# Loading three tiles' keys and queries in 32x32 squares and turning them on VectorE instead of TensorE

## The chip, the cores and the metric

One NeuronCore of a Trainium2 chip runs the whole program in one launch. The metric is the device time of one execution in microseconds (us), and the median of three runs stands for a kernel. The engines are TensorE (PE in the profile, its weight loads PEld), VectorE (DVE), ScalarE (ACT), GpSimd (POOL) and SyncE (SP), which here only issues DMAs. Each engine runs its own instruction list in order, and semaphores order the engines among each other.

## The reference: windowed attention, then two feed-forward stages

```python
# q, k, v: [2, 8, 768, 64] float32; sinks 4, window 128
scores = scale * q @ k.T; keep = (pos_k < 4) | (0 <= pos_q - pos_k < 128)
a = softmax(where(keep, scores, -1e9)); x = (a @ v) -> [1536, 512]
out = sum_e p[:, e] * (relu(x @ w1[e]) @ w2[e])   # 4 experts, F = 1024
h = out @ w_in; return (h * cos(h)) @ w_out       # d_ff = 2048
```

## The kernel before

The 1536 tokens are 12 tiles of 128 (`T` = 12, 6 for each batch), and the 8 heads make 4 pairs for each tile. The attention stage runs in rounds `i` = 0 to 26. Round `i` computes the scores of two head pairs, so tile `t` has its scores in rounds 2t and 2t+1. Each engine has its own loop over the rounds, written by hand, and that order is the order of its instructions. In round `i`:

- PE computes the scores of the round (`scores`, L1406), turns the weights of the round before (`turn_weights`, L1417), turns keys or queries of a tile that is needed later (`turn_keys` L1349 in odd rounds, `turn_queries` L1368 in even ones, four 128x128 transposes against the identity each), turns the sink weights with the sums (`turn_sinks` L1382, odd rounds) and multiplies weights with values three rounds late (`weigh_values` L1441, `weigh_sinks` L1455).
- DVE merges and masks the scores (`merge` L1042, `mask_head` L1058), copies turned keys out of PSUM (`copy_keys` L1069), for three tiles the queries too (`copy_queries` L1075, the tiles in `QUERIES_BY_DVE`), inverts the sums (L1087, L1091), and in rounds 18, 20, 21 and 23 makes one of four sums of the first batch's result for the feed-forward stage (`sum_tokens` L1129).
- ACT takes the exponentials (L779), copies turned weights (L787), the other tiles' queries (`copy_queries` L796) and the result (`copy_out` L768).
- POOL splits the sink weights (`gather_sinks`, L610 and L612, even rounds), parts the turned weights (`part_weights`, L595 and L598), copies sink keys (L630), makes low halves of expert weights (`first_lo` L665, in rounds 11, 13 and 15) and multiplies the result of tile `t` with its norms in round 2t+6 (`normalise` L651).
- SP has a loop over tiles, `t` = 1 to 12: two norm DMAs for tile t-3, keys of tile t+3, the store of tile t-2's inverse sums, queries of tile t+3, values of tile t. The norm DMAs read back, spread over 64 partitions each, what the store wrote (`load_norm` L436).

PE may be one pair ahead of the masks: `scores(j)` waits until the pair j-2 is masked. `turn_sinks(t)` waits for `gather_sinks(t)`, and `scores` of a tile waits for its keys and queries in `k_t` and `q_t`. From round 24 on the feed-forward products follow (three matmuls in fp32r for each fp32 product), some 750 us of them; they start when the masks are done and the first tokens are split. `turn_squares` (L1264) and `place_squares` (L472) of that stage already turn tiles with VectorE and small DMAs.

## Time and profile before

| | |
|---|---|
| median of 3 runs | 837.62 us (834.06 to 837.65) |
| profiled execution | 837.64 us, span 835.9 us |
| PE, DVE, ACT, POOL busy | 831.0, 455.7, 458.0, 551.7 us |
| granted TensorE clock | 1.00 in all 40 slices |
| DMA packets | 101045, 70.46 MB, 68368 of them under 512 B |

The profile is one execution. The span is what the engines' records cover, and the execution's own time is 1.7 us more. A busy PE is not a PE at its peak, since the ends of matmuls are modelled. In a timeline each row is a start, a length, and what ran; a bracket gives the idle time before it and who ended it.

### The profile page before, as it was taken

The numbers are of one execution on the slowest core, as the hardware profiler recorded it, in microseconds if no ns is written. First come the engines' busy times: TensorE is split into PE (matmuls) and PEld (weight loads), VectorE is DVE, ScalarE is ACT, GpSimd is POOL, SyncE is SP. The second block draws the span as 40 slices with busy tenths as digits, with TensorE's granted clock in tenths as the row PEclk, the third lists the DMA queues.
The fourth block names the chain that finished last, engine by engine and source line by source line (L and its number), as shares of the span: only waits on it lengthen the run. The fifth ranks groups of instructions, "written<-read, shape, count | busy, mean of one in ns | idle before, by whom it ended". The sixth has DMA issues, their size and how long they took to land.

```text
span 835.9 us, 13778 instructions
## 1 busy us (share of the span) xinstructions
PE 831.0 (99%) x4564; PEld 743.6 (89%) x4564; DVE 455.7 (55%) x947; ACT 458.0 (55%) x985; POOL 551.7 (66%) x417
## 2 busy tenths in 40 slices
PE   9999999999999999999999999999999999999998
PEld 7777989988988988988988998998998998998997
DVE  4988833523523427633433433338767749756756
ACT  5888734334334435433423523525867869867864
POOL 3777996476476778575475575878384399685450
PEclk9999999999999999999999999999999999999999
DMA  8785231211221220432331131130223430530202
GB/s 184 169 190 147 67 123 51 102 61 44 98 68 44 91 83 19 117 105 53 95 112 50 52 101 51 51 101 30 73 63 76 125 117 0 177 102 18 84 1 76
DMA packets 101045, 70.46 MB, mean 84 GB/s; under 512 B 68368, under 2 KB 74864, under 8 KB 100976
## 3 DMA queue, kind: packets, MB, share of 16 engines
q1 hardware_dynamic: 100976, 69.58, 28.5%
q8 instruction: 39, 0.64, 0.3%
q14 instruction: 30, 0.25, 0.1%
HBM read 62.96 MB, written 3.19 MB: 79 GB/s over the span
## 4 chain that ended last, share of the span: by engine, by line
PE 96%; DVE 1%; issue 1%; ACT 1%; DMA 0%; SPq 0%; ACTq 0%; DVEq 0%
PE scores L1499 11%; PE scores L1503 11%; PE scores L1501 11%; PE scores L1512 10%; PE scores L1514 10%; PE scores L1510 10%; PE bank L1512 5%; PE bank L1514 5%; PE bank L1510 5%; PE bank L1499 3%; PE bank L1501 3%; PE bank L1503 3%; PE scores L1406 2%; PE bank L1441 2%; PE bank L1417 1%
## 5 line engine op out<-in xcount | busy, mean ns | idle before, releaser
L665 POOL TENSOR_TENSOR w_lo<-w_raw,w_hi 128x512 fp32r<-128x512 f32 x96 | 129.8, 1362 | 139.0 <-ACT w_hi L814 139.0
L1499 PE MATMUL scores<-x_hi,w_hi 128*128 128x384 f32 x528 | 177.1, 335 | 0.4 <-DVE x_lo L1136 0.2
L1503 PE MATMUL scores<-x_hi,w_lo 128*128 128x384 f32 x528 | 176.8, 335 | 0.0
L1501 PE MATMUL scores<-x_lo,w_hi 128*128 128x384 f32 x528 | 176.5, 334 | 0.0
L672 POOL TENSOR_TENSOR w_lo<-w_raw,w_hi 128x1024 fp32r<-128x1024 f32 x48 | 116.2, 2431 | 65.4 <-ACT w_hi L824 65.4
L824 ACT ACTIVATE w_hi<-w_raw 128x1024 fp32r<-128x1024 f32 x48 | 50.9, 1060 | 190.2 <-PE scores L1514 188.8
L1514 PE MATMUL scores<-w_hi,h_lo 128*128 128x512 f32 x384 | 149.3, 389 | 0.0
L1512 PE MATMUL scores<-w_lo,h_hi 128*128 128x512 f32 x384 | 149.3, 389 | 0.0
L1510 PE MATMUL scores<-w_hi,h_hi 128*128 128x512 f32 x384 | 149.0, 388 | 0.0
L1240 DVE SCALAR_TENSOR_TENSOR acc<-scores,probs,acc 128x512 f32<-128x512 f32 x56 | 41.8, 749 | 116.5 <-PE scores L1514 116.5
L1499 PEld LDWEIGHTS scores<-x_hi,w_hi 128*128 128x128 f32 x528 | 99.1, 188 | 2.4 <-issue 0.7
L1501 PEld LDWEIGHTS scores<-x_lo,w_hi 128*128 128x128 f32 x528 | 99.1, 188 | 0.9
L1503 PEld LDWEIGHTS scores<-x_hi,w_lo 128*128 128x128 f32 x528 | 99.1, 188 | 0.0
L665 POOL TENSOR_TENSOR w_lo<-w_sum,w_hi 128x768 fp32r<-128x768 f32 x48 | 92.5, 1928 | 0.0
L1514 PEld LDWEIGHTS scores<-w_hi,h_lo 128*128 128x128 f32 x384 | 72.1, 188 | 14.9
L1510 PEld LDWEIGHTS scores<-w_hi,h_hi 128*128 128x128 f32 x384 | 72.1, 188 | 14.1
L1512 PEld LDWEIGHTS scores<-w_lo,h_hi 128*128 128x128 f32 x384 | 72.1, 188 | 14.0
L1512 PE MATMUL bank<-w_lo,h_hi 128*128 128x512 f32 (+1 forms) x196 | 76.0, 388 | 0.0
L1514 PE MATMUL bank<-w_hi,h_lo 128*128 128x512 f32 (+1 forms) x196 | 75.9, 387 | 0.0
L1510 PE MATMUL bank<-w_hi,h_hi 128*128 128x512 f32 (+1 forms) x196 | 75.8, 387 | 0.0
L660 POOL TENSOR_TENSOR w_sum<-w_raw 128x512 f32<-128x512 f32 x46 | 59.5, 1293 | 15.8 <-DMA w_raw<-in_moe_w_in_dram 13.6
L1204 DVE SCALAR_TENSOR_TENSOR h_lo<-scores,h_hi 128x384 fp32r<-128x384 f32 x64 | 35.5, 554 | 44.1 <-ACT h_hi L878 42.6
(140 smaller groups left out, 1548.0 us busy)
## 6 DMA issues: line engine op xcount, KB each, us to landing
w_raw<-in_moe_w_dram SPq DMA_DIRECT2D x30, 1024.0 KB, 5.1
w_raw<-in_moe_w_in_dram SPq DMA_DIRECT2D x8, 1024.0 KB, 5.0
w_raw<-in_moe_w_out_dram SPq DMA_DIRECT2D x8, 1024.0 KB, 5.4
v_nat<-in_v_dram SPq DMA_DIRECT2D x12, 256.0 KB, 4.0
norm<-routing_dram SPq DMA_DIRECT2D x24, 128.0 KB, 3.2
x_t<-t_sum SPq DMA_DIRECT2D x192, 16.0 KB, 1.9
k_nat<-in_k_dram SPq DMA_DIRECT2D x11, 256.0 KB, 3.8
q_nat<-in_q_dram SPq DMA_DIRECT2D x11, 256.0 KB, 3.6
```

The lines of the kernel that those rows point to most:

```text
L660: nc.gpsimd.tensor_tensor(*weight_sum(n)).then_inc(w1_summed, 1)
L665: nc.gpsimd.tensor_tensor(w1_slots(w1_lo, h % 2, part), w1_part(h % 2, part), w1_slots(w1_hi, h % 2, part).bitcast(F32), ALU.subtract)\
L672: nc.gpsimd.tensor_tensor(w2_lo[:, i::2], w2_raw[:, i::2], w2_hi[:, i::2].bitcast(F32), ALU.subtract)\
L824: nc.scalar.activation(w2_hi[:, i::2], w2_raw[:, i::2], ACT.Copy).then_inc(w2_hi_ready, 1)
L1204: nc.vector.scalar_tensor_tensor(h_part(h_lo, h % 2, c), c_source(h % 2, c), 0.0, h_part(h_hi, h % 2, c).bitcast(F32), ALU.max, ALU.subtract)\
L1240: kept_one = nc.vector.scalar_tensor_tensor(acc[:, n], down_bank[k][:], probs[:, n, e:e + 1], acc[:, n], ALU.mult, ALU.add)
L1499: nc.tensor.matmul(target[:, 0:HALF], w1_hi[:, i, slot, d], x_hi[:, n - 1, d], start=first and d == 0, stop=False, skip_group_check=True)
L1501: nc.tensor.matmul(target[:, 0:HALF], w1_hi[:, i, slot, d], x_lo[:, n - 1, d], start=False, stop=False, skip_group_check=True)
L1503: last = nc.tensor.matmul(target[:, 0:HALF], w1_lo[:, i, slot, d], x_hi[:, n - 1, d], start=False, stop=d == 1, skip_group_check=True)
L1510: nc.tensor.matmul(target[:, cols], h_hi[:, i, f, toks], w2_hi[:, c, cols], start=i == 0 and f == 0, stop=False, skip_group_check=True)
L1512: nc.tensor.matmul(target[:, cols], h_hi[:, i, f, toks], w2_lo[:, c, cols], start=False, stop=False, skip_group_check=True)
L1514: return nc.tensor.matmul(target[:, cols], h_lo[:, i, f, toks], w2_hi[:, c, cols], start=False, stop=i == 1 and f == 1, skip_group_check=True)
```

## The change

- The keys and queries of tiles 9, 10 and 11 (`SQUARED` = 9) are no longer loaded as rows and turned by PE. 16 DMAs for keys and 16 for queries (`load_squares`), each of 32 partitions with 12 runs of 32 floats (48 KB), put the 32x32 squares where a square-by-square turn on DVE leaves the wanted layout. Keys go to `k_squares`, a part of `x_t` that is not in use yet, queries to `q_squares`, which lies under `x_lo`. One semaphore counts all 16 DMAs of each, so the first turned tile waits for all of them.
- DVE turns them with one `transpose` for each tile and kind, at the places in its loop where it copied them, in rounds 15 to 20. PE loses `turn_keys` and `turn_queries` of these tiles.
- The queries of tile 1 are copied by DVE instead of ACT.
- The sums 0 and 1 of the first batch are made by POOL in rounds 17 and 19 instead of DVE in rounds 18 and 20.
- The inverse sums are kept in another order of heads (`sum_at`), so that each norm DMA reads 64 x 512 floats in one run for each partition instead of four runs.

```diff
-QUERIES_BY_DVE = (7, 8, 9)
+QUERIES_BY_DVE = (1, 7, 8)
...
+        def sum_at(h):
+            return h % 2 * PAIRS + h // 2
...
+            def load_squares(dst, src, first, last, signal):
+                for n in range(first, last):
+                    h, f = divmod(n, 2)
+                    p, r = divmod(h, 2)
+                    rows = slice((2 * r + f) * 32, (2 * r + f + 1) * 32)
+                    source = src[1, h, (SQUARED - TPB) * P:S, f * 32:(f + 1) * 32]
+                    sp.dma_start(dst[rows, p, :].rearrange("j (c i) -> j c i", i=32),
+                                 source.rearrange("(c j) i -> j c i", j=32)).then_inc(signal, 16)
...
-                if 5 <= t + 3 < T:
+                if 5 <= t + 3 < SQUARED:
                     load_keys(t + 3)
                 if t >= 2:
                     store_inverse(t - 2)
-                if 5 <= t + 3 < T:
+                if 5 <= t + 3 < SQUARED:
                     load_queries(t + 3)
                 if 3 <= t < T:
                     load_values(t)
+                if t == 2:
+                    load_squares(k_squares, k, 0, 4, k_squares_landed)
+                elif t == 3:
+                    load_squares(k_squares, k, 4, 10, k_squares_landed)
+                elif t == 4:
+                    load_squares(k_squares, k, 10, 16, k_squares_landed)
+                elif t == 5:
+                    load_squares(q_squares, q, 0, 6, q_squares_landed)
+                elif t == 6:
+                    load_squares(q_squares, q, 6, 12, q_squares_landed)
+                elif t == 7:
+                    load_squares(q_squares, q, 12, 16, q_squares_landed)
...
+                if i in (17, 19):
+                    sum_tokens(0, (17, 19).index(i))
...
+                    nc.vector.transpose(target, k_squares[:, :, n * P:(n + 1) * P]).then_inc(k_ready, 1)
...
+            def turn_queries(t):
+                dve.wait_ge(q_squares_landed, 16 * SQUARE_PARTS)
+                dve.wait_ge(scores_done, PAIRS * (t - 1))
+                n = t - SQUARED
+                nc.vector.transpose(q_t[:, t % 2], q_squares[:, :, n * P:(n + 1) * P]).then_inc(q_squares_ready, 1)
...
-                if i % 2 == 1 and (i + 3) // 2 < T:
+                if i % 2 == 1 and (i + 3) // 2 < SQUARED:
                     turn_keys((i + 3) // 2)
-                elif i >= 2 and i % 2 == 0 and i // 2 + 1 < T:
+                elif i >= 2 and i % 2 == 0 and i // 2 + 1 < SQUARED:
                     turn_queries(i // 2 + 1)
```

SP in its loop for tiles 5 and 6, before. L436 are the norm DMAs, L410, L428, L416 and L422 the keys, the inverse sums, the queries and the values:

```order
L436 DMA norm<-routing_dram 64x4x128 x2
L410 DMA k_nat<-in_k_dram 128x8x64
L428 DMA routing_dram<-inverse 8x128
L416 DMA q_nat<-in_q_dram 128x8x64
L422 DMA v_nat<-in_v_dram 128x8x64
```

The same five of the changed kernel (L466, L429, L457, L435, L451), with the squares behind them (L445):

```order
L466 DMA norm<-routing_dram 64x512 x2
L429 DMA k_nat<-in_k_dram 128x8x64
L457 DMA routing_dram<-inverse 8x128
L435 DMA q_nat<-in_q_dram 128x8x64
L451 DMA v_nat<-in_v_dram 128x8x64
L445 DMA x_t<-in_k_dram 32x12x32 x6
```

Each SP loop from tile 3 to tile 6 has six more DMAs between the values and the norms of the next one; tiles 2 and 7 have four more.

PE in rounds 15 and 16, before, from the turned weights of round 15 to the values of round 16 (L1349 turns the keys of tile 9, L1368 its queries):

```order
L1417 MATMUL bank<-ident,weights 128x128 x4
L1349 MATMUL bank<-ident,k_nat 128x128 x4
L1382 MATMUL bank<-ident,sink_w 8x128
L1441 MATMUL bank<-weights_t,v_nat 64x128 x4
L1406 MATMUL scores<-k_t,q_t 128x264 x4
L1417 MATMUL bank<-ident,weights 128x128 x4
L1368 MATMUL bank<-ident,q_nat 128x128 x4
L1441 MATMUL bank<-weights_t,v_nat 64x128 x4
```

The changed kernel there:

```order
L1479 MATMUL bank<-ident,weights 128x128 x4
L1441 MATMUL bank<-ident,sink_w 8x128
L1503 MATMUL bank<-weights_t,v_nat 64x128 x4
L1468 MATMUL scores<-k_t,q_t 128x264 x4
L1479 MATMUL bank<-ident,weights 128x128 x4
L1503 MATMUL bank<-weights_t,v_nat 64x128 x4
```

One group of four transposes is gone from each of the rounds 15 to 20.

DVE behind the masks of round 18, before: the sums' inversion and the first token sum (L1129):

```order
L1058 ISA neg_max 128x1
L1087 TENSOR_TENSOR row_sum<-row_sum,tiny 128x8
L1091 RECIPROCAL sink_w<-row_sum 128x8
L1129 TENSOR_TENSOR t_sum<-x_t 128x768
L1042 COPY_PREDICATED scores<-in_prev,scores 128x2x128
```

The changed kernel there, with the turn of tile 10's queries (L1132) ahead of the inversion:

```order
L1097 ISA neg_max 128x1
L1132 STREAM_TRANSPOSE q_t<-q_squares 128x512
L1143 TENSOR_TENSOR row_sum<-row_sum,tiny 128x8
L1147 RECIPROCAL sink_w<-row_sum 128x8
L1081 COPY_PREDICATED scores<-in_prev,scores 128x2x128
```

The token sum has left DVE's rounds 18 and 20, and a transpose has come in.

## Rows read from the trace of the kernel before

**Rows 1.** The page: the chain that ended last, by engine.

```profile
PE 96%; DVE 1%; issue 1%; ACT 1%; DMA 0%; SPq 0%; ACTq 0%; DVEq 0%
```

**Rows 2.** Stages: stretch, its length, busy PE, PEld, DVE, ACT, POOL; clock, DMA share, GB/s.

```profile
60.00:76.00 16.00, 16.00 (x162) 12.46 (x161) 13.96 (x64) 14.48 (x52) 12.58 (x22) 1.00 0.54 141
...
33.00:40.00 7.00, 7.00 (x75) 5.50 (x71) 6.49 (x28) 5.60 (x21) 6.91 (x10) 1.00 1.00 219
```

**Rows 3.** Timeline of PE: scores of rounds 17, 18, 21 (L1406), `turn_sinks(7)` (L1382).

```profile
61.03 1.16 PE L1406 MATMUL scores<-k_t,q_t 64*128 64x264 f32 x8
...
63.05 0.27 PE L1382 MATMUL bank<-ident,sink_w 128*104 128x128 f32 x1
...
64.28 1.16 PE L1406 MATMUL scores<-k_t,q_t 64*128 64x264 f32 x8
...
74.60 1.16 PE L1406 MATMUL scores<-k_t,q_t 64*128 64x264 f32 x8
```

**Rows 4.** The chain in order of time: start, us on the chain.

```profile
72.81 0.44 PE bank L1368 x4
```

**Rows 5.** Timeline of DVE, rounds 16 to 21.

```profile
59.09 0.43 DVE L1042 COPY_PREDICATED scores<-in_prev,scores 128x256 f32<-128x256 int32 x1
...
60.89 0.69 DVE L1075 COPY q_t<-bank 128x512 f32<-128x512 f32 x1
...
61.82 0.41 DVE L1042 COPY_PREDICATED scores<-in_prev,scores 128x256 f32<-128x256 int32 x1
...
65.04 0.43 DVE L1042 COPY_PREDICATED scores<-in_prev,scores 128x256 f32<-128x256 int32 x1 [0.24 <-PE scores L1406]
...
67.16 0.91 DVE L1129 TENSOR_TENSOR t_sum<-x_t 128x768 f32<-128x768 f32 x1
68.58 0.43 DVE L1042 COPY_PREDICATED scores<-in_prev,scores 128x256 f32<-128x256 int32 x1 [0.52 <-PE scores L1406]
...
75.37 0.43 DVE L1042 COPY_PREDICATED scores<-in_prev,scores 128x256 f32<-128x256 int32 x1 [0.52 <-PE scores L1406]
```

**Rows 6.** Groups of DVE after 130 us, shapes apart: the transposes.

```profile
L1264 DVE STREAM_TRANSPOSE t_sum<-acc 128x512 f32<-128x512 f32 x12 | 7.8, 686 | 0.0
```

**Rows 7.** Timeline of SP's queue: start, time that the issue took.

```profile
17.67 2.04 SPq L443 DMA_DIRECT2D w_raw<-in_moe_w_dram  x4
...
26.26 0.39 SPq L416 DMA_DIRECT2D q_nat<-in_q_dram  x1
...
29.78 1.62 SPq L410 DMA_DIRECT2D k_nat<-in_k_dram  x1
31.45 0.48 SPq L428 DMA_DIRECT2D routing_dram<-inverse  x1
...
35.46 0.60 SPq L410 DMA_DIRECT2D k_nat<-in_k_dram  x1
...
51.04 1.24 SPq L436 DMA_DIRECT2D norm<-routing_dram  x2
...
61.14 0.40 SPq L422 DMA_DIRECT2D v_nat<-in_v_dram  x1
...
341.36 20.66 SPq L472 DMA_DIRECT2D x_t<-t_sum  x32
```

**Rows 8.** DMA issues by tile: count, KB each, median us to landing.

```profile
norm<-routing_dram SPq DMA_DIRECT2D x24, 128.0 KB, 3.2
x_t<-t_sum SPq DMA_DIRECT2D x192, 16.0 KB, 1.9
```

**Rows 9.** Timeline of POOL, rounds 14 to 16: `normalise(4)`, `part_weights(14)`, `gather_sinks(7)`.

```profile
55.30 1.27 POOL L651 TENSOR_TENSOR x_t<-x_t,norm 128x512 f32<-128x512 f32 x1 [1.62 <-DMA norm<-routing_dram]
58.52 0.64 POOL L595 TENSOR_SCALAR_AFFINE_SELECT weights_t<-weights_t 128x512 f32<-128x512 f32 x1 [1.96 <-ACT weights_t L787]
...
61.06 0.24 POOL L610 CAST sink_w<-weights 128x64 fp32r<-128x64 f32 x1
61.39 0.25 POOL L612 TENSOR_TENSOR sink_w<-weights,sink_w 128x32 fp32r<-128x32 f32 x1
```

More of the change, by code:

```diff
@@ L51, in program @@
     ROUNDS = ND + VALUE_LAG
+    SQUARED = T - 3
+    SQUARE_PARTS = 2 * H
     KC = DM // P
@@ L110, in program @@
         x_hi = sb("x_hi", [P, 7, 2, HALF], F32R)
+        early = ExitStack()
+        sb("early_lo", [P, 2, 2, HALF], stack=early)
+        q_squares = sb("q_squares", [P, PAIRS, HALF], stack=early)
+        early.close()
         x_lo = sb("x_lo", [P, 7, 2, HALF], F32R)
@@ L300, in sums_in_memory @@
             at = t % TPB * rows
-            return routing[at:at + rows, :].rearrange("(p r s) e -> p r (s e)", p=PAIRS, r=2)
+            return routing[at:at + rows, :].rearrange("(h s) e -> h (s e)", h=H)
         def weights_of(s):
@@ L434, in load_norm @@
                     sp.wait_ge(x_ready, t - 1)
+                sums = sums_in_memory(t).rearrange("(r p) s -> r (p s)", r=2)
                 for r in range(2):
-                    sp.dma_start(norm[r * D:(r + 1) * D, t % 2],
-                                 sums_in_memory(t)[:, r].unsqueeze(0).broadcast_to([D, PAIRS, P]))\
-                        .then_inc(norm_landed[t % 2], 16)
+                    sp.dma_start(norm[r * D:(r + 1) * D, t % 2].rearrange("d p s -> d (p s)"),
+                                 sums[r].unsqueeze(0).broadcast_to([D, PAIRS * P])).then_inc(norm_landed[t % 2], 16)
             def load_parts(dst, n, first, signal):
@@ L792, in copy_queries @@
                 act.wait_ge(q_turned, t + 1)
-                if t >= 2:
-                    act.wait_ge(scores_done, PAIRS * (t - 1))
-                source = out_bank if t == 1 else turn_bank
-                nc.scalar.activation(q_t[:, t % 2], source[:].rearrange("p (k s) -> p k s", k=PAIRS), ACT.Copy)\
+                act.wait_ge(scores_done, PAIRS * (t - 1))
+                nc.scalar.activation(q_t[:, t % 2], turn_bank[:].rearrange("p (k s) -> p k s", k=PAIRS), ACT.Copy)\
                     .then_inc(q_ready, 1)
@@ L923, in _ @@
                     exp_head(i, 3)
-                if i >= 2 and i % 2 == 0 and i // 2 + 1 < T and i // 2 + 1 not in QUERIES_BY_DVE:
+                if i >= 2 and i % 2 == 0 and i // 2 + 1 < SQUARED and i // 2 + 1 not in QUERIES_BY_DVE:
                     copy_queries(i // 2 + 1)
@@ L1063, in copy_keys @@
             def copy_keys(t):
-                dve.wait_ge(k_turned, t + 1)
+                if t < SQUARED:
+                    dve.wait_ge(k_turned, t + 1)
+                else:
+                    dve.wait_ge(k_squares_landed, 16 * SQUARE_PARTS)
                 if t >= 3:
@@ L1068, in copy_keys @@
                     dve.wait_ge(k_sink_kept, (t - 3) // TPB + 1)
[L1069 to L1070 removed]
+                target = k_t[:, :, t % 3, 0:P]
+                if t < SQUARED:
+                    nc.vector.tensor_copy(target, turn_bank[:].rearrange("p (k s) -> p k s", k=PAIRS))\
+                        .then_inc(k_ready, 1)
+                else:
+                    n = t - SQUARED
+                    nc.vector.transpose(target, k_squares[:, :, n * P:(n + 1) * P]).then_inc(k_ready, 1)
             def copy_queries(t):
                 dve.wait_ge(q_turned, t + 1)
+                if t >= 2:
+                    dve.wait_ge(scores_done, PAIRS * (t - 1))
+                source = out_bank if t == 1 else turn_bank
+                nc.vector.tensor_copy(q_t[:, t % 2], source[:].rearrange("p (k s) -> p k s", k=PAIRS))\
+                    .then_inc(q_ready, 1)
+            def turn_queries(t):
+                dve.wait_ge(q_squares_landed, 16 * SQUARE_PARTS)
                 dve.wait_ge(scores_done, PAIRS * (t - 1))
[L1075 to L1076 removed]
+                n = t - SQUARED
+                nc.vector.transpose(q_t[:, t % 2], q_squares[:, :, n * P:(n + 1) * P]).then_inc(q_squares_ready, 1)
             def copy_sinks(t):
@@ L1123, in sum_tokens @@
             def sum_tokens(n):
-                if n == 0:
-                    dve.wait_ge(x_ready, TPB)
-                else:
-                    dve.wait_ge(x_summed, n)
+                dve.wait_ge(x_summed, n)
                 nc.vector.tensor_tensor(*token_sum(0, n)).then_inc(x_summed, 1)
@@ L1150, in _ @@
                     copy_keys(1)
+                if i == 1:
+                    copy_queries(1)
                 if i % 2 == 1 and (i + 3) // 2 < T:
                     copy_keys((i + 3) // 2)
-                elif i % 2 == 0 and i // 2 + 1 in QUERIES_BY_DVE:
+                elif i >= 2 and i % 2 == 0 and i // 2 + 1 in QUERIES_BY_DVE:
                     copy_queries(i // 2 + 1)
+                elif i % 2 == 0 and SQUARED <= i // 2 + 1 < T:
+                    turn_queries(i // 2 + 1)
                 if i % 2 == 0 and 0 <= (i - 2) // 2 < T:
@@ L1165, in _ @@
                     sum_weights(i - 7)
-                if i in (18, 20, 21, 23):
-                    sum_tokens((18, 20, 21, 23).index(i))
+                if i == 21:
+                    sum_tokens(2)
+                elif i == 23:
+                    sum_tokens(3)
                 if i == 22:
@@ L1390, in scores @@
                 else:
-                    pe.wait_ge(q_ready, t)
+                    if t < SQUARED:
+                        pe.wait_ge(q_ready, t)
+                    else:
+                        pe.wait_ge(q_squares_ready, t - SQUARED + 1)
                     pe.wait_ge(k_ready, t)
```

14 lines of the change are left out of this document (6 added, 8 removed).

## The prediction

> **What bounds the kernel now.** I read the chain that ended last first: 96% of it is PE [rows 1], so time is saved only where PE, or what PE waits for, gets shorter. The 750 us of products are not touched. What changes lies in the attention stage, before about 88 us, so I read its stages next. From 60 to 76 us PE is busy for 16.00 of 16 us, but DVE for 13.96 and ACT for 14.48 [rows 2]: three engines run nearly level, and taking work from one of them soon meets the next. The timelines show who leads. PE goes from the scores of round 17 (61.03) to those of round 21 (74.60) without a wait, 13.57 us for four rounds [rows 3]. DVE in the same rounds waits for PE's scores: 0.24 us before round 18, 0.52 before round 19, and the same two waits again before rounds 20 and 21, 1.52 us in all [rows 5]. So PE leads with a margin of 1.5 us over DVE in four rounds, and no more.
>
> **What PE loses.** Four transposes take 0.44 us on the chain [rows 4]. Six such groups go, in rounds 15 to 20: 2.64 us, if nothing else becomes the limit.
>
> **What DVE gets.** The nearest row of a DVE transpose is 686 ns for 128x512 floats from SBUF to SBUF [rows 6], and the copy out of PSUM that it replaces takes 0.69 [rows 5]. Keys of three tiles and queries of tile 9 are therefore swapped at no cost. Queries of tiles 10 and 11 come new, and two token sums of 0.91 us leave. Round by round: the even round 16 of before already has a queries' operation and no sum, and runs from 59.09 to 61.82, 2.73 us; the odd round 17 runs from 61.82 to 65.04 less the wait of 0.24, 2.98 us [rows 5]. All rounds of the changed kernel from 16 to 20 look like these two: 2.73 + 2.98 + 2.73 + 2.98 + 2.73 = 14.15 us. From 59.09 that ends at 73.24, where before round 21 began at 75.37: 2.1 us earlier. PE alone would give 2.64; the smaller number holds, since PE can be only one pair ahead of the masks. Behind round 21 DVE's list is unchanged and was already without a gap, so what is won or lost at the start of round 21 stays to the end. The ceiling of the change is 2.1 us.
>
> **What SP gets.** 32 DMAs more, 6 fewer. The trace has no load into 32 partitions in runs of 128 B. The nearest row is `place_squares`, also 32 partitions and runs of 128 B: 32 issues in 20.66 us, 0.646 each. The other bound is the weight loads, 4 in 2.04 us, 0.51 each [rows 7]. I take 0.646, by shape. The rest of one loop, each with a gap of 0.05: norms 1.29, keys 0.65, store 0.53, queries 0.44, values 0.45 [rows 7], together 3.36 us. Six squares make it 7.24, more than the 6.8 us that two rounds of PE take (13.57 / 2). Here SP stops being a queue with slack. By hand from the end of the queries of tile 5 at 26.65: four squares to 29.2; three loops (tiles 3, 4, 5) of 7.24 to 51.0; tile 6 without keys and queries, 2.27 + 3.88, to 57.1; tile 7, 2.27 + 2.58, to 62.0, with the last issue at 61.4. Landing takes 1.9 us for the small squares inside SBUF and 3.2 for the norms, which come from HBM [rows 8]: 63.3 to 64.6.
>
> The new wait: `turn_queries(9)` on DVE stands where the copy stood, at 60.89 [rows 5], since round 16 starts no earlier than before. It waits for all 16 query squares, 2.4 to 3.7 us. Behind it on DVE are the inversion and the masks of round 17, and behind those PE's scores of round 18. Nothing covers it: DVE has no gap there. Less the 2.1 won, that is 0.3 to 1.6 us lost.
>
> The norms lie behind the same squares. Before, `normalise(4)` already waited 1.62 us for its norm and began at 55.30 [rows 9]. Now the norms of tile 4 are issued at 57.1 and 57.8 and land 3.2 later, at 61.0. On POOL, `normalise(4)` (1.25), `part_weights(14)` to `gather_sinks(7)` (58.52 to 61.64, 3.12 us [rows 9]) follow in order, so the sinks of tile 7 are ready at 65.4. PE wants them in `turn_sinks(7)`, at 63.05 before [rows 3]. The scores of round 18 come 1.23 later, at 66.6, and those of round 21 after 10.32 us less three groups of 0.44, 9.0: 75.6 against 74.60 [rows 3]. That is 1.0 us late. Both chains run side by side and agree: the first in its middle and the second each give about 1.0 us lost.
>
> The keys' squares are issued by 43.7 and wanted after 58: covered. The wider norm runs save POOL nothing; if an issue were as cheap as a weight load (0.51 for 0.62) they would give SP 0.2 us for each loop. I take nothing and keep it for the range. DMA share is 1.00 from 33 to 40 us [rows 2], with six more DMAs to come there: landings can only get longer.
>
> The Trainium skill speaks against this change: "DMA: Bandwidth & Descriptors", section "Rules for kernel authors", says to coalesce many small transfers into one large one, because under 64 KB mostly overhead is paid; these are 48 KB each. The issue row of `place_squares` agrees, 0.65 us for 16 KB against 0.60 for the keys' 256 KB. By the row, the 32 squares take 20.7 us of SP, and the sum is the one below; by the page the queue would be paid by the number of transfers and not by bytes, which gives the same 838.6.
>
> **POOL's two sums.** Each is a 128x768 operation. From 58.52 to 61.06 POOL does two selects of 0.64 and `first_lo` with 128x512 [rows 9], so that one takes at most 1.26, and a 768 wide one at most 1.9. They stand in rounds 17 and 19, where POOL waited; the parted weights are wanted three rounds later. I cost them at nothing; if POOL is late already, the first delays `gather_sinks(8)` and each us of it is one of PE's. Queries of tile 1 move to DVE at 11 us, where it waits for PE: nothing.
>
> The Trainium skill, "SBUF — State Buffer", section "SBUF: two separate sides", says that a DVE operation with two SBUF inputs and a GpSimd operation hold their shared port pair exclusively, the other blocking for the whole instruction. By that, moving sums off DVE also spares POOL's selects some blocking; no run shown here isolates it, and no term of the sum rests on it.
>
> **Sum.** 837.64 (the profiled execution, 0.02 over the median of the runs) + 1.0 = 838.6.
>
> **Rivals.**
> 1. *The squares are cheap and all land in time.* At 0.51 for each the same chain by hand reads 28.7, 47.9, 53.3 and 57.6, and the last squares land from 59.0 to 60.3, before 60.89. Then the ceiling holds: 837.64 - 2.1 = 835.5. For it: the row of weight loads. Against: all rows with fewer than 128 partitions lie at 0.6 or above. The stall begins at 0.55 for each (41.3 us of other issues and the start, plus 32 of them, plus a landing of 2.5 in the middle); at 0.62 gain and stall cancel.
> 2. *Back-pressure on SP makes it much later.* Before, one keys issue took 1.62 us instead of 0.60 [rows 7]; the DMA engines are full at 33 to 40 us. If some 2.5 us of such delays fall into three loops that no longer have waits to swallow them, both chains end 2.5 later: 837.64 + 1.0 + 2.5 = 841.1. This is the rival on the slow side; it decides from the first keys issue over 1.5 us.
> 3. *The change doesn't get to the end.* POOL's or ACT's list before the first products eats the gain: 837.6, inside the first forecast's own range.
>
> **How the numbers follow.** SP late by about what is won, 837.0 to 839.8: 0.45 (rival 3 with it). In time, 834.8 to 837.0: 0.30. Much later, 839.8 to 842: 0.20. Anything else 0.05. The range from 835.0 to 841.3 leaves 2 in 10 out. A measurement of this kernel tells about 0.5% (4.2 us) from no change. Faster than 833.4 needs more than the ceiling: 0.03. Slower than 841.8: 0.06. Within: 0.91.
>
> **What would show it.** PE has no transposes of keys in rounds 15 to 20. DVE's transposes take 0.69. SP's issues of squares take 0.6 to 0.65, and its loops for tiles 3 to 5 have no wait. DVE waits 2 to 4 us for `q_squares` before the first transpose of queries; POOL waits for norms in rounds 10 to 16, and PE at `turn_sinks` in rounds 13 or 17. If DVE doesn't wait there, rival 1 holds. The prediction is wrong if DVE's transposes take another time, or if the products after 88 us run otherwise.

## The result, and the profile after

The changed kernel takes 839.88 us (median of 6 runs, 838.58 to 841.5), the kernel before 835.18 us (6 runs beside them, 834.06 to 837.65): ratio 1.0056, 95% interval 1.0037 to 1.0074. It is slower by about 4.7 us (3.1 to 6.2). The two profiled executions stand at 837.64 and 841.5 us, spans 835.9 and 839.7. One of the four times of `a_loads_only` was disturbed (1523.69 us, at a granted clock of 0.80) and is left out everywhere. The page's chain by engine and line, of the changed kernel:

```profile
PE 93%; DVE 3%; issue 1%; SPq 1%; DMA 1%; ACT 0%; POOL 0%; DVEq 0%; ACTq 0%; POOLq 0%
```

PE had 96% of it before [rows 1]. DVE has 3% now, and SP's queue and DMA have appeared. The stages of the changed kernel (stretch, its length, busy PE, PEld, DVE, ACT, POOL; clock, DMA share, GB/s):

```profile
47.00:54.00 7.00, 4.88 (x55) 4.02 (x53) 5.02 (x23) 6.27 (x23) 4.92 (x9) 1.00 0.90 184
54.00:60.00 6.00, 6.00 (x54) 4.56 (x50) 3.16 (x15) 2.25 (x9) 2.53 (x4) 0.72 0.63 134
60.00:76.00 16.00, 14.74 (x139) 10.19 (x139) 14.65 (x64) 13.21 (x49) 13.75 (x20) 1.00 0.63 154
```

From 60 to 76 us PE was busy for 16.00 us before [rows 2] and is for 14.74 now. Part of that is the work that was taken away, part is waiting, and the real loss lies ahead of it: 2.1 us of PE's time are gone in 47:54, and in 54:60 the clock is granted at 0.72, with PE busy all the time and every other engine short of work. PE's timeline in that place (L1441 `turn_sinks`, L1503 values, L1468 scores, L1479 turned weights, L1561 first product):

```profile
45.21 0.29 PE L1441 MATMUL bank<-ident,sink_w 128*104 128x128 f32 x1 [0.67 <-POOL sink_w L653]
...
53.47 0.29 PE L1441 MATMUL bank<-ident,sink_w 128*104 128x128 f32 x1 [1.89 <-POOL sink_w L653]
53.69 1.25 PE L1503 MATMUL bank<-weights_t,v_nat 128*64 128x128 f32 x16
54.87 2.13 PE L1468 MATMUL scores<-k_t,q_t 64*128 64x264 f32 x8
56.93 1.11 PE L1479 MATMUL bank<-ident,weights 128*128 128x128 f32 x4
...
59.83 1.16 PE L1468 MATMUL scores<-k_t,q_t 64*128 64x264 f32 x8
...
64.76 1.16 PE L1468 MATMUL scores<-k_t,q_t 64*128 64x264 f32 x8
...
67.43 0.29 PE L1441 MATMUL bank<-ident,sink_w 128*104 128x128 f32 x1 [0.61 <-POOL sink_w L653]
...
78.29 1.16 PE L1468 MATMUL scores<-k_t,q_t 64*128 64x264 f32 x8
...
87.80 0.45 PE L1561 MATMUL scores<-x_hi,w_hi 128*128 128x384 f32 x1
```

The kernel before has no wait there, and its rounds 14 and 15 and its first product begin at

```profile
51.98 1.16 PE L1406 MATMUL scores<-k_t,q_t 64*128 64x264 f32 x8
...
55.52 1.16 PE L1406 MATMUL scores<-k_t,q_t 64*128 64x264 f32 x8
...
83.94 0.44 PE L1499 MATMUL scores<-x_hi,w_hi 128*128 128x384 f32 x1
```

Read it as a ledger against before. Round 17's scores began at 61.03 [rows 3] and begin at 64.76, 3.73 us late; round 21's 74.60 has become 78.29, 3.69 late; and the first product comes 3.86 late, which is the difference of the spans (3.8). So everything was lost before round 17. Two pieces make most of it; a third, the wait of 0.67 at `turn_sinks(4)`, is nearly outweighed by the transposes that PE no longer has in rounds 15 and 16. The wait of 1.89 us at `turn_sinks(5)` is the first. The clock is the second: it ran at the lower of its two levels (1.2 and 2.4 GHz) for a part of 54:60: the scores of round 14, 1.16 us long in other rounds, take 2.13, and the turned weights 1.11 in place of 0.66. Round 14 lasts 4.96 us (54.87 to 59.83), where it took 3.54 before (51.98 to 55.52): 1.4 us. SP's queue shows where the wait comes from (start, time that the issues took):

```profile
36.71 1.12 SPq L466 DMA_DIRECT2D norm<-routing_dram  x2
...
40.58 4.59 SPq L445 DMA_DIRECT2D x_t<-in_k_dram  x6
45.30 1.10 SPq L466 DMA_DIRECT2D norm<-routing_dram  x2
...
52.91 1.09 SPq L466 DMA_DIRECT2D norm<-routing_dram  x2
...
61.47 2.10 SPq L445 DMA_DIRECT2D q_squares<-in_q_dram  x4
```

Up to there the norms are issued every 8.6 us, while two rounds of PE take 6.8. Those of tile 2 leave at 45.30, 5.2 us later than before, where they left at

```profile
40.14 1.24 SPq L436 DMA_DIRECT2D norm<-routing_dram  x2
```

POOL waits for them, and the sinks' weights stand behind `normalise(2)` in its list:

```profile
49.00 1.27 POOL L692 TENSOR_TENSOR x_t<-x_t,norm 128x512 f32<-128x512 f32 x1 [2.77 <-DMA norm<-routing_dram]
...
51.55 1.26 POOL L706 TENSOR_TENSOR w_lo<-w_raw,w_hi 128x512 fp32r<-128x512 f32 x1
52.76 0.24 POOL L651 CAST sink_w<-weights 128x64 fp32r<-128x64 f32 x1
53.07 0.25 POOL L653 TENSOR_TENSOR sink_w<-weights,sink_w 128x32 fp32r<-128x32 f32 x1
```

The last row ends at 53.3, and PE goes on at 53.47. DVE's first transpose of queries had next to no wait, and each transpose takes 0.71 us where 686 ns [rows 6] was costed:

```profile
65.29 0.71 DVE L1132 STREAM_TRANSPOSE q_t<-q_squares 128x512 f32<-128x512 f32 x1 [0.25 <-DMA q_squares<-in_q_dram]
```

DMA issues of the changed kernel (count, KB each, median us to landing):

```profile
norm<-routing_dram SPq DMA_DIRECT2D x24, 128.0 KB, 2.9
...
x_t<-in_k_dram SPq DMA_DIRECT2D x16, 48.0 KB, 2.2
q_squares<-in_q_dram SPq DMA_DIRECT2D x16, 48.0 KB, 2.3
```

Once issued, a square or a norm lands sooner than the norms did before (3.2 [rows 8], with shorter runs). They are not slow; they are late to start.

**Two courses of the start.** The times fall into two groups: of 35 runs of the kernel before in one set, 26 lie from 833.4 to 835.5 us and 9 from 837.3 to 838.8. The traces show two kinds of start. The same turn of keys in the changed kernel and, below it, in `d_sums_dve` (an experiment below):

```profile
8.34 1.06 PE L1408 MATMUL bank<-ident,k_nat 128*128 128x128 f32 x4
```

```profile
7.45 0.61 PE L1407 MATMUL bank<-ident,k_nat 128*128 128x128 f32 x4
```

In the profiled executions of the kernel before and of the changed one, matmuls have the long duration until about 13 us; in those of the eleven experiments whose profiles are read below, until about 7 us, and round 3 begins at 11.8 to 12.7 us in place of 15.7 to 15.9. The clock column reads 1.00 in all of them. That the start makes the two groups is inferred from the size. It follows that the two profiles above may be compared with each other, and that the 837.64 on which the prediction was built lies in the upper group.

### The profile page after: what moved, and what is told of

The parts are those of the page before. It is cut to its first block, busy times and chain, and to the rows that moved or that the text cites. A ratio compares the mean times of both kernels' runs of the same rounds, so it can differ in the third digit from the quotient of the medians.

```text
span 839.7 us, 13751 instructions
## 1 busy us (share of the span) xinstructions
PE 830.8 (99%) x4540; PEld 741.9 (88%) x4540; DVE 459.3 (55%) x948; ACT 456.3 (54%) x982; POOL 553.7 (66%) x419
## 4 chain that ended last, share of the span: by engine, by line
PE 93%; DVE 3%; issue 1%; SPq 1%; DMA 1%; ACT 0%; POOL 0%; DVEq 0%; ACTq 0%; POOLq 0%
PE scores L1561 11%; PE scores L1565 11%; PE scores L1563 11%; PE scores L1576 10%; PE scores L1574 10%; PE scores L1572 10%; PE bank L1574 5%; PE bank L1576 5%; PE bank L1572 5%; PE bank L1561 3%; PE bank L1563 3%; PE bank L1565 3%; PE scores L1468 1%; PE bank L1503 1%; DVE scores L1081 1%
## 5 line engine op out<-in xcount | busy, mean ns | idle before, releaser
L1561 PE MATMUL scores<-x_hi,w_hi 128*128 128x384 f32 x528 | 177.1, 335 | 0.4 <-DVE x_lo L1189 0.2
L1561 PEld LDWEIGHTS scores<-x_hi,w_hi 128*128 128x128 f32 x528 | 99.1, 188 | 2.4 <-issue 0.7
```

What stands on the lines that cost most here:

```text
L1561: nc.tensor.matmul(target[:, 0:HALF], w1_hi[:, i, slot, d], x_hi[:, n - 1, d], start=first and d == 0, stop=False, skip_group_check=True)
```

## The experiments

Each ratio is against runs of the kernel before in the same set on the same chip; the sets differ in their base (834.3 to 835.2 us), so that kernels of two sets are best compared by their ratios. "First product" is where L1561 or its like begins in the profiled execution; what follows it takes 751.9 to 752.1 us in every kernel, so that this one number carries the whole difference. The profiled executions below `after` all started early. Their first products are to be read against the 80.87 of `j_before_late`, which is the kernel before with one operation of POOL a round later, and not against 83.94. PE's waits are those for the sinks' weights, POOL's those for norms, each of 0.25 us or more.

| run | median us | ratio (interval) | first product | PE's waits | POOL's |
|---|---|---|---|---|---|
| before (late start) | 835.18 | 1 | 83.94 | none | 4.6 |
| after (late start) | 839.88 | 1.0056 (1.0037 to 1.0074) | 87.80 | 3.2 | 13.2 |
| a_loads_only | 846.04 | 1.0142 (1.0127 to 1.0157) | | | |
| b_no_loads | 833.15 | 0.9989 (0.9978 to 1.0001) | 77.93 | none | 3.9 |
| c_norm_between | 840.94 | 1.0073 (1.0060 to 1.0086) | 88.66 | 3.9 | 10.3 |
| d_sums_dve | 841.86 | 1.0093 (1.0078 to 1.0108) | 88.87 | 4.1 | 10.3, and 4.7 for ACT |
| e_twelfth | 837.53 | 1.0026 (1.0011 to 1.0041) | 83.86 | 3.3 | 12.4 |
| f_long_runs | 838.04 | 1.0039 (1.0023 to 1.0055) | 83.94 | 4.6 | 13.3 |
| g_key_loads | 838.07 | 1.0029 (1.0011 to 1.0047) | 84.17 | 3.5 | 9.3 |
| h_no_squares | 834.72 | 0.9996 (0.9979 to 1.0012) | 81.62 | 1.2 | 6.2 |
| i_late_normalise | 840.89 | 1.0073 (1.0054 to 1.0091) | 85.36 | 3.7 | 6.8 |
| j_before_late | 835.15 | 1.0013 (1.0000 to 1.0025) | 80.87 | none | 0.9 |
| k_by_act | 835.90 | 1.0013 (1.0000 to 1.0027) | 82.09 | 1.4 | 8.6 |
| l_both_queues | 834.71 | 0.9991 (0.9978 to 1.0004) | 81.39 | 1.4 | 9.9 |

The theory after the result: the 32 loads cost the time, and they cost it through SP's queue. The rivals: the loads cost it in the DMA engines (many short runs); POOL's new sums or the order of its work cost it; the transposes on DVE cost it.

### The loads alone, and the change without them

`a_loads_only` is the kernel before with

```diff
+                if t == 2:
+                    load_squares(k_squares, k, 0, 4, k_squares_landed)
+                ...                      # as in the change, up to t == 7; nobody reads the squares
```

> The kernel before, with the 32 loads of squares added to SP at the places of the changed kernel, and nobody reading them; all other work stays as it was. Theory (the squares' issues on SP make the norms late, POOL waits for them, and PE waits for POOL in turn_sinks): PE waits 0.5 us or more at turn_sinks(4) and 1.5 us or more at turn_sinks(5), and the kernel is 4 to 8 us slower than before, more than the changed kernel, since keys and queries of the last tiles are loaded too. Rival (POOL's two sums and DVE's extra transposes cost the time): within 1 us of before.

Measured: 1.0142, some 12 us, more than the 4 to 8 expected. The loads are added to the keys' and queries' own loads here, not put in their place. No profile of it is read, so the waits that were expected at `turn_sinks(4)` and `turn_sinks(5)` are not shown for this kernel.

```diff
-                if t == 2:
-                    load_squares(k_squares, k, 0, 4, k_squares_landed)
-                ...
+            nc.vector.memset(k_squares, 0.0)
+            nc.vector.memset(q_squares[:], 0.0)
```

> The changed kernel without the 32 loads of squares; the squares are filled with zeros by two memsets on DVE ahead of the first masks, so keys and queries of the last three tiles are zeros. Everything else of the change stays. Theory (late norms): no wait at turn_sinks, and 1.5 to 2.2 us faster than before, the ceiling of the prediction. Rival (POOL's sums slow DVE's small operations and PE's rounds 17 to 21 gain nothing): 0 to 1 us faster than before, with rounds 17 to 21 at 13.5 us as before.

Measured: 0.9989, the fastest median of all, and less than was expected (1.5 to 2.2 us faster). The median hides part of it: seven of its twelve times lie from 831.5 to 833.3 us and five from 835.2 to 835.6, while the 17 times of the kernel before beside them lie in one group, from 833.7 to 835.5. The median of the lower seven, 832.06, is 2.3 us under the 834.34 of before. In `b_no_loads` the scores of rounds 15, 17 and 21 begin at

```profile
51.59 1.16 PE L1457 MATMUL scores<-k_t,q_t 64*128 64x264 f32 x8
...
56.52 1.16 PE L1457 MATMUL scores<-k_t,q_t 64*128 64x264 f32 x8
...
68.65 1.16 PE L1457 MATMUL scores<-k_t,q_t 64*128 64x264 f32 x8
```

The first of the six groups of transposes stood behind the scores of round 15, and the last ahead of those of round 21. Between these two, `b_no_loads` takes 17.06 us and the kernel before 19.08 (55.52 to 74.60): 2.02 us won, 1.44 of them behind the scores of round 17. The turn on DVE does what it should, and the loads take back all of it and more. The norms of tile 2 leave at 35.67 here, where the other early start without squares, `j_before_late`, has them at 36.29:

```profile
35.67 1.10 SPq L466 DMA_DIRECT2D norm<-routing_dram  x2
```

### The other two edits

`d_sums_dve` gives both sums back to DVE:

```diff
-                if i in (17, 19):                       # POOL
-                    sum_tokens(0, (17, 19).index(i))
-                if i == 21: ...                         # DVE
+                if i in (18, 20, 21, 23):
+                    sum_tokens((18, 20, 21, 23).index(i))
```

> The changed kernel with the two token sums back on DVE in rounds 18 and 20. Theory (late norms are the cost; the sums matter little): 0 to 1.5 us slower than the changed kernel, by two sums of 0.9 us on a DVE without gaps. Rival (POOL's sums are the cost, by their 1.8 us each and by slowing DVE's small operations of two SBUF inputs): 1 us or more faster than the changed kernel.

Measured: 1.0093, some 3 us slower by the two ratios than with the sums on POOL, where 0 to 1.5 were expected; the rival (faster) falls. PE's waits at the sinks stay, and small ones for DVE come new. The wait of POOL ahead of the 3.11, 4.75 us, is put down to ACT's copy of the result, which ended at 48.12; the norms had been issued from 43.70 on, so by the landing time of 2.9 both came at nearly the same moment (an estimate):

```profile
52.69 0.42 PE L1440 MATMUL bank<-ident,sink_w 128*104 128x128 f32 x1 [3.11 <-POOL sink_w L653]
54.95 2.13 PE L1467 MATMUL scores<-k_t,q_t 64*128 64x264 f32 x8
...
74.20 0.71 PE L1467 MATMUL scores<-k_t,q_t 64*128 64x264 f32 x4 [0.32 <-DVE neg_max L1095]
```

`h_no_squares` is the kernel before with the wider norm runs and the two sums on POOL, no squares:

```diff
+                sums = sums_in_memory(t).rearrange("(r p) s -> r (p s)", r=2)
+                if i in (17, 19):                       # POOL
+                    sum_tokens(0, (17, 19).index(i))
```

> The kernel before with the two other edits of the change and no squares: row sums stored in the order that gives the norm DMAs runs of 2 KB, and the first two token sums on POOL. My theory: both are worth nothing by themselves or a few tenths, since POOL's waits for norms in the kernel before hold nobody and PE sets the end: ratio 0.998 to 1.000. Rival: the sums on POOL stretch VectorE's small operations in rounds 17 to 20 and delay normalise, ratio 1.001 to 1.003; PE would then wait for masked or for sinks in rounds 18 to 21.

Measured: 0.9996 (0.9979 to 1.0012). Both edits together are worth nothing that can be measured. POOL waits 5.31 us for the first norm here, and PE 1.20 behind it for the sinks of tile 3; `j_before_late` has no such wait of PE, and what makes it stays open. With `d_sums_dve`, where taking the sums off POOL gained nothing, this rules out POOL's sums as the cause of the 5 us.

### Issues or bytes

`e_twelfth` keeps the 32 issues and cuts each to one block of twelve, 4 KB in place of 48:

```diff
-                    source = src[1, h, (SQUARED - TPB) * P:S, f * 32:(f + 1) * 32]
-                    sp.dma_start(dst[rows, p, :].rearrange("j (c i) -> j c i", i=32),
-                                 source.rearrange("(c j) i -> j c i", j=32)).then_inc(signal, 16)
+                    source = src[1, h, (SQUARED - TPB) * P:(SQUARED - TPB) * P + 32, f * 32:(f + 1) * 32]
+                    sp.dma_start(dst[rows, p, 0:32], source).then_inc(signal, 16)
```

> The changed kernel with the same 32 square DMAs in the same places of SP's queue, but each carries only one 32x32 block (4 KB) in place of twelve (48 KB); the rest of both square buffers is zeroed at the start by VectorE, so keys and queries of the last three tiles are mostly zero. It keeps SP's 32 issues and takes 11/12 of the bytes and short runs from the DMA engines. Theory 1 (the DMA engines are full with short runs, and so the norms and the issues themselves are late): SP issues a square in about 0.55 us, SP's queue is 17 to 18 us longer in place of 21.9, the norms land nearly as in the kernel without the loads, PE waits at most 0.5 us for the sinks' weights, no fall of the clock; ratio to the kernel before 0.998 to 1.001. Theory 2 (the 32 issues in SP's queue are what makes the norms late): norms issued as late as in the changed kernel to within 1 us, POOL waits over 9 us for them, PE waits over 2 us at the turns of sinks, ratio 1.003 to 1.007.

Measured: 1.0026, between the two expectations in time, and by theory 2 in the trace. SP and PE in `e_twelfth`:

```profile
42.03 1.10 SPq L465 DMA_DIRECT2D norm<-routing_dram  x2
...
45.87 3.20 SPq L445 DMA_DIRECT2D q_squares<-in_q_dram  x6
```

```profile
50.99 0.43 PE L1442 MATMUL bank<-ident,sink_w 128*104 128x128 f32 x1 [2.75 <-POOL sink_w L652]
...
53.25 1.67 PE L1469 MATMUL scores<-k_t,q_t 64*128 64x264 f32 x8
```

Six issues take 3.2 us, 0.53 each, though they carry 4 KB. The wait of PE is there with its clock fall (0.78 in 47:54), and the first product comes 5.9 us later than in `b_no_loads`. By the ratios to 0.9989 it keeps 0.0037 of 0.0067. So a twelfth of the bytes keeps more than half of the harm, and the rest is not explained by the count of issues alone. My number for theory 1 (1.001 at most) fell with it.

`f_long_runs` keeps bytes and issues and doubles the run:

```diff
-                    source = src[1, h, (SQUARED - TPB) * P:S, f * 32:(f + 1) * 32]
-                    sp.dma_start(dst[rows, p, :].rearrange("j (c i) -> j c i", i=32),
+                    at = (SQUARED - TPB) * P + f * 192
+                    source = src[1, h, at:at + 192, :]    # 64 floats in a run
+                    sp.dma_start(dst[rows, p, :].rearrange("j (c i) -> j c i", i=64),
```

> The changed kernel with the same 32 square DMAs, the same bytes and the same partitions, but each reads 64 elements in a run (256 bytes, half the tokens of both halves of a head) in place of 32 (128 bytes); the blocks land in other places, so keys and queries of the last three tiles hold wrong numbers. It halves the number of runs. Theory 1 (short runs fill the DMA engines): the DMA share in 33:60 falls by about a tenth, an issue of a square takes 0.55 to 0.6 us, POOL's waits for the norms fall from 13.2 us to 8 to 10, ratio to the kernel before 1.000 to 1.004. Theory 2 (SP's issues alone): nothing moves, ratio 1.005 to 1.008, POOL's waits over 12 us.

Measured: 1.0039, between again. The DMA share in 33:60 falls from 0.76 to 0.67, as theory 1 has it, and an issue of a square takes 0.65 in the mean; POOL's waits stay at 13.3 us, as theory 2 has it, and PE waits 4.6 us for the sinks, no less than in the changed kernel. What differs is the clock. Behind a wait of 2.54 us it does not fall here:

```profile
50.27 0.29 PE L1442 MATMUL bank<-ident,sink_w 128*104 128x128 f32 x1 [2.54 <-POOL sink_w L654]
...
51.52 1.16 PE L1469 MATMUL scores<-k_t,q_t 64*128 64x264 f32 x8
```

In eight of the twelve executions of `f_long_runs`, and of `e_twelfth`, the granted clock of the whole was 1.00; in all six of the changed kernel it was 0.998. So part of what these two kernels save may be the fall that most of their executions lack (1.4 us in the changed kernel), and not runs or bytes. The length of a run is at most a small part; against the changed kernel's 1.0056, in another set of runs, the intervals overlap.

`g_key_loads` leaves out the 16 loads of queries:

```diff
-                elif t == 5:
-                    load_squares(q_squares, q, 0, 6, q_squares_landed)
-                ...                                      # and t == 6, t == 7
```

> The changed kernel with the 16 loads of key squares and without the 16 of query squares (that buffer is zeroed, so queries of the last three tiles are zero). The waits of PE at the turns of sinks stand at 45.2, 53.5 and 67.4 in the changed kernel: the first two while or just after the key squares are issued (26 to 45) and the first query squares (48.9). If each norm is late by the squares issued ahead of it in the same loops: norms of tiles 0 to 2 as in the changed kernel, PE's wait near 45 stays (0.5 to 0.9), the one at 53.5 shrinks to under 1, no fall of the clock; ratio to the kernel before 1.000 to 1.003. If instead the sum of all 32 counts only through the last norms (tiles 3 to 5), the ratio is at or below 0.999.

Measured: 1.0029, and my forecast for the waits was wrong. I expected the one near 53 to shrink to under 1 us; it came at 51.49 with 3.12 us and a granted clock of 0.82. The 16 issues of keys alone make the norms of tile 2 leave at 42.66 and give half of the loss. The clock's fall has a price here that the times show: the four of twelve executions with a granted clock of 1.00 took 835.2 to 835.9 us, the eight with less 837.7 to 840.2 (late starts may be among these). Half the loads do not give half the waits: by these waits, what counts is how long SP's loop is while the norms of tiles 1 and 2 pass through it.

### Moving the waiting elsewhere

`c_norm_between` puts the norms in the middle of each loop's squares:

```diff
+                    load_squares(dst, src, first, middle, signal)
+                    load_norm(t - 2)
+                    load_squares(dst, src, middle, last, signal)
```

> The changed kernel with the norm DMAs of tiles 0 to 5 moved ahead on SP, into the middle of the squares of the loop before (three squares, two norms, three squares). The same DMAs, the same bytes. Theory (order on SP's queue): POOL waits for norms less than half as long (10.9 us in the changed kernel), no wait at turn_sinks over 0.5 us, 2 to 4 us faster than the changed kernel. Rival (the DMA engines are full, so all transfers are late whatever their order): the norms land as late as in the changed kernel and the time is within 1 us of it.

Measured: 1.0073, no better. `i_late_normalise` lets POOL ask for the norm one round later:

```diff
-                if i % 2 == 0 and 0 <= (i - 6) // 2 < T - 4:
-                    normalise((i - 6) // 2)
+                if i % 2 == 1 and 0 <= (i - 7) // 2 < T - 4:
+                    normalise((i - 7) // 2)
```

> The changed kernel with one edit on POOL: each product x times norm of tiles 0 to 7 stands one round later, behind POOL's other work of that round, so that it waits for its norm when the preparation of the sinks' weights is no longer queued behind 4 us of other work. Nothing else moves; SP's queue is that of the changed kernel. Theory A (SP's queue of 32 issues is longer than the rounds it serves, and whoever meets its result first waits): PE's waits for sink_w fall under 1 us in sum, but the last query squares then come too late and VectorE waits 2 to 4 us for q_squares near 60 us, as it did when the norms stood between the squares; ratio to the kernel before 1.002 to 1.006. Theory B (only the order on POOL costs, and the loads are covered once it is mended): no wait of VectorE over 1 us, ratio 0.998 to 1.000.

Measured: 1.0073, by theory A, though a little above its range. Of `i_late_normalise`, DVE and then PE:

```profile
62.22 0.71 DVE L1132 STREAM_TRANSPOSE q_t<-q_squares 128x512 f32<-128x512 f32 x1 [2.88 <-DMA q_squares<-in_q_dram]
```

```profile
63.32 0.29 PE L1441 MATMUL bank<-ident,sink_w 128*104 128x128 f32 x1 [2.21 <-DVE sink_w L1147]
```

PE's waits for POOL's part of the sinks shrink to 1.4 us in sum (under 1 was expected), and DVE's wait for the query squares, the one that the prediction put first, appears with 2.88 us. In `c_norm_between` it is 2.85, with PE waiting 2.77 behind it. PE also waits for values, whose DMAs stand in the same queue: 0.97 and 1.02 us in `i_late_normalise`, 0.34 and 0.81 in `c_norm_between`. Each cure hands the delay to the next in line, because SP's queue stays as long as it was. The control:

```diff
+                if i % 2 == 1 and 0 <= (i - 7) // 2 < T - 4:   # in the kernel before
+                    normalise((i - 7) // 2)
```

> The kernel before with the same edit on POOL alone (product x times norm one round later), as the control. The profiled execution of the kernel before has no wait of PE for sink_w over 0.3 us, so both theories: no difference, ratio 0.998 to 1.001; if it were faster by 1 us or more, part of a gain of the edit in the changed kernel is not to be put down to the squares.

Measured: 1.0013 (1.0000 to 1.0025), at most a small loss; the edit by itself gains nothing.

### The same loads from another queue

`k_by_act` issues all 32 from ScalarE, two or three in each of rounds 3 to 14; bytes, runs and places stay:

```diff
-                    sp.dma_start(dst[rows, p, :]...
+                    nc.scalar.dma_start(dst[rows, p, :]...
```

> The changed kernel with the 32 square DMAs issued from ScalarE's queue, two or three in each of rounds 3 to 14, in place of SP's. Same bytes and runs. Theory 1 (SP's queue carries the delay): norms issued as in the kernel without the loads, POOL's waits for norms fall to 4 to 6 us, no wait of PE for sink_w over 0.5 us. But ScalarE is 80 to 90% busy in 26:54 of the changed kernel and each issue takes it 0.55 to 0.65 us, 1.6 us a round against about 0.5 us that it has free: PE waits for ScalarE's weights instead, 0.5 to 1 us a round over twelve rounds, and the ratio is 1.005 to 1.015. Theory 2 (the DMA engines alone): the norms stay late, POOL's waits over 10 us; ratio 1.005 or more as well, but with the waits of the changed kernel. A ratio under 1.001 would say that ScalarE's issues cost it nothing, and that another queue is the whole cure.

Measured: 1.0013, under the range of both theories. Theory 1 holds in the main and not in its figures: the norms are issued 4.8 to 6.9 us apart and no longer 8.6, but those of tile 2 leave at 39.96, 4.3 later than in `b_no_loads`; POOL's waits are 8.6 us (4 to 6 expected), 6.1 of them for the first norm, and PE waits once for the sinks, 1.35 (0.5 at most expected). My price for ScalarE was too high: the first issue of each round takes it 0.32 to 0.40 us, those behind it 0.49 to 1.03, and PE waits 2.6 us for ScalarE's results in all, against 0.7 in `b_no_loads`. Windows of `k_by_act`:

```profile
26.00:60.00 34.00, 31.20 (x315) 23.95 (x311) 27.71 (x122) 25.87 (x96) 23.21 (x35) 1.00 0.95 181
```

The same window of the changed kernel:

```profile
26.00:60.00 34.00, 31.21 (x310) 24.61 (x308) 28.10 (x118) 24.43 (x91) 21.24 (x36) 0.95 0.77 163
```

The DMA engines are busier (0.95 against 0.77) and the kernel is faster by 3.6 us by the two ratios. That rules out the bytes as the main cause.

`l_both_queues` divides the issues, half from each engine:

```diff
+                    counts = (0, 2, 5, 8, 11, 14, 16)      # SP, loops 2 to 7: f = 0
+                    for m in range(4 * (i - 3) // 3, 4 * (i - 2) // 3):   # ScalarE, rounds 3 to 14: f = 1
```

> The changed kernel with half of the 32 square DMAs (two or three for each of the six loops) in SP's queue and the other half in ScalarE's queue, one or two in each of rounds 3 to 14. Same bytes and runs. By the dose seen so far (all 32 on SP 1.0056 to 1.0073, all on ScalarE 1.0013, none 0.9989) and since SP's loop with three more issues (1.7 us on some 3.7) again fits the 6.8 us of two rounds: norms issued at most 1 us later than without the loads, VectorE's wait for q_squares under 1 us, PE's waits for sink_w under 1 us in sum, ratio 0.999 to 1.002, near or under the one with ScalarE alone. If the bytes and short runs in the DMA engines were what is left of the cost, it stays at 1.001 to 1.003 however the issues are divided; if it were ScalarE's issue time, it falls to 0.999 to 1.000.

Measured: 0.9991 (0.9978 to 1.0004), 834.71 against 835.18. SP and PE of `l_both_queues`:

```profile
41.07 1.95 SPq L466 DMA_DIRECT2D norm<-routing_dram  x2
...
48.22 1.09 SPq L466 DMA_DIRECT2D norm<-routing_dram  x2
```

```profile
36.71 0.29 PE L1452 MATMUL bank<-ident,sink_w 128*104 128x128 f32 x1 [1.06 <-POOL sink_w L648]
...
50.19 0.29 PE L1452 MATMUL bank<-ident,sink_w 128*104 128x128 f32 x1 [0.36 <-POOL sink_w L648]
```

The norms leave at most 7.15 us apart and catch up, no clock falls, DVE doesn't wait for squares, and all of the 5 us are back. Two of the forecasts missed: the norms of tile 2 leave 5.4 us later than in `b_no_loads` (41.07 against 35.67), not 1, and PE's waits for the sinks are 1.4 us, not under 1. It is as fast as the kernel before, within what can be measured, and not faster: the 2 us won by the turn are spent ahead of round 15, whose scores begin at 54.97 here and at 52.31 in `j_before_late`. How much of that is due to ScalarE's issues is not shown; the wait of 1.06 behind a late first norm is one that `h_no_squares` has without any square (1.20). No version here that computes the right result beats the kernel before.

## Why the prediction was right or wrong

The predicted 838.6 lies 1.3 us under the measured 839.88, and 839.88 lies in the range. That is luck, for two errors cancel: the base was too high and the step too small. The prediction was "profiled execution before + 1.0", with 837.64 taken as the kernel before; further runs put its median at 834.3 to 835.2. The step to compare is the +1.0, and it measured +3.9 between the two profiles of like start and +4.7 between the medians. It was the right sign and the right cause at a quarter of the size or less.

- *PE's gain 2.64, held to 2.1.* Right in size: `b_no_loads` wins 2.02 us from the scores of round 15 to those of round 21, and 2.08 to the first product. That DVE is what holds it is not shown, since the only waits of PE over 0.2 us there are two for ScalarE's weights, 0.22 and 0.24. In the changed kernel rounds 17 to 21 take 13.53 us against 13.57, no gain, since they include the wait of 0.61 and start with everybody late.
- *An issue of a square takes 0.646.* Right in the mean: 32 took 21.9 us, 0.68 each, from 0.53 with nothing in the way to 0.83.
- *SP's loop of 7.24 us, longer than 6.8.* Right as the cause, mis-sized: the norms left 8.6 us apart, since values issues took up to 1.08 in place of 0.40 and squares up to 0.83. The last squares of loops 6 and 7 were issued 1.6 to 2.1 us later than the hand chain had them.
- *DVE waits 2.4 to 3.7 us for the query squares.* It waited 0.25, because PE and DVE had already been held up by more than that. In `c_norm_between` and `i_late_normalise`, where less held them up, it waited 2.85 and 2.88. The wait was real, and second in line. The prediction's own sign (if DVE doesn't wait there, the squares are cheap and in time) would have pointed to the wrong rival.
- *The norms hold POOL, POOL holds `turn_sinks(7)`, 1.0 us lost.* This is the step that failed, and by its extent: I followed one norm, that of tile 4, and took those before it to be covered. With loops 1.8 us too long from tile 3 on, the norms of tile 2 were 5.2 us late already, and `turn_sinks(5)` waited 1.89 us, four rounds ahead of the place that I had worked out. Its round, 13, is named among the signs to look for, but has no price in the sum.
- *A wait costs its own length.* Not foreseen: the clock fell behind the wait of 1.89 and made round 14 longer by 1.4 us.
- *POOL's sums and the wider norm runs at nothing.* Right within what `h_no_squares` can tell (0.9979 to 1.0012); the sums took 1.82 each, as the bound of 1.9 had it.
- *The keys' squares are covered.* Right for their landing, and wrong as a way to put it: their issues were what delayed the norms (`g_key_loads`, 1.0029 by them alone).

Rival 1 (squares cheap) fell. Rival 2 (back-pressure, 841.1) came nearest: it stands 3.5 us over its base, where 3.9 were measured, and its time is 1.2 off; its trigger (a keys issue over 1.5 us) didn't happen behind the first squares, where keys took 0.59, but squares and values were stretched. The Trainium skill's rule that was weighed is to coalesce many small transfers ("DMA: Bandwidth & Descriptors", "Rules for kernel authors"). It speaks of a transfer's own overhead, not of the queue that issues it; by that rule `e_twelfth` agrees for the queue too: the issue was paid by the count, 0.53 us at 4 KB as at 48 where nothing stood in the way.

Open: how the 2.5 us between the ratios of `e_twelfth` and the changed kernel divide among bytes, run length, falls of the clock and chance; the sets of runs differ and the intervals touch.

## What to carry to other kernels

A small DMA is paid on the queue that issues it, and the one who pays is whatever stands behind it in that queue: add up the issues of one turn of the loop, and if they exceed the time of the rounds that it serves, follow the first victim, since the delay grows with each turn. Here moving the waiting instruction, or the norms within the queue, only handed the delay on; another queue, or dividing the issues over two, removed most or all of it. Compare profiles only when they started alike, and take the base from several runs.

## What the runs showed of the hardware

The clock fell after some waits of PE, not after all: after 1.89 us in the changed kernel (0.72 granted in the next 6 us), 3.11 and 2.75 in `d_sums_dve` and `e_twelfth`, 3.12 in `g_key_loads`, even after two of 0.76 and 0.81 within 2 us in `c_norm_between` (scores of 1.92 us behind them), but not after 2.21 in `i_late_normalise` and 2.54 in `f_long_runs`, where the scores behind them took 1.29 and 1.16. So the length of the last wait alone doesn't tell, and executions of one kernel differ (four of twelve of `g_key_loads` without a fall).

A tiny operation of DVE with two inputs in SBUF ends with POOL's. DVE in the changed kernel, 0.16 us long when alone:

```profile
49.14 1.16 DVE L1143 TENSOR_TENSOR row_sum<-row_sum,tiny 128x8 f32<-128x8 f32 x1
...
65.92 0.87 DVE L1143 TENSOR_TENSOR row_sum<-row_sum,tiny 128x8 f32<-128x8 f32 x1
...
72.38 0.76 DVE L1143 TENSOR_TENSOR row_sum<-row_sum,tiny 128x8 f32<-128x8 f32 x1
```

POOL in the same places (its first is the 49.00 above):

```profile
65.50 1.27 POOL L706 TENSOR_TENSOR w_lo<-w_raw,w_hi 128x512 fp32r<-128x512 f32 x1
...
71.30 1.82 POOL L731 TENSOR_TENSOR t_sum<-x_t 128x768 f32<-128x768 f32 x1
```

DVE's ends are 50.30, 66.79 and 73.14, POOL's 50.27, 66.77 and 73.12. The Trainium skill ("SBUF — State Buffer", "SBUF: two separate sides") says that such a pair of operations excludes each other for the whole instruction; by that, the trace agrees.
